# Mask rows for each bit of a hash, made by GpSimd; scores capped in place with their minimum

## What is computed

```python
q_bits = (np.einsum('bhsd,dk->bhsk', q, proj) > 0)      # 6 bits per row
k_bits = (np.einsum('bhsd,dk->bhsk', k, proj) > 0)
mask = q_bucket[:, :, :, None] == k_bucket[:, :, None, :]
scores = np.where(mask, scale * np.matmul(q, k.transpose(0, 1, 3, 2)), -1000000000.0)
attn = np.exp(scores - np.max(scores, axis=-1, keepdims=True))
attn = attn / (np.sum(attn, axis=-1, keepdims=True) + 1e-09)
out = np.matmul(attn, v)
```

## Time and profile before

| what | value |
|---|---|
| median of the runs | 616.49 us (616.34 to 616.92) |
| profiled execution | 616.41 us |
| its span in the trace | 614.7 us |
| TensorE busy | 605.4 us, 98% of the span |
| VectorE busy | 431.1 us, 70% |
| ScalarE busy | 347.6 us, 57% |
| GpSimd busy | 349.3 us, 57% |

### The profile page before, as it was taken

How to read it: one execution, slowest core, us unless ns; L and a number is a source line. 1 busy time by engine, 2 the same in 40 slices (tenths; PEclk the granted TensorE clock), 3 DMA queues, 4 the chain that set the end, 5 groups by cost and what they waited for, 6 DMA issues and landing times.

```text
span 614.7 us, 10917 instructions
## 1 busy us (share of the span) xinstructions
PE 605.4 (98%) x3676; PEld 503.5 (82%) x3676; DVE 431.1 (70%) x689; ACT 347.6 (57%) x700; POOL 349.3 (57%) x337
## 2 busy tenths in 40 slices
PE   7899999999999999999999999999999999999998
PEld 3667777776776776999888999999999999988887
DVE  3988888888888885788676666545677666579920
ACT  3877777777777785354444444335444444264232
POOL 4533434333337756146458988873999999234140
PEclk9999999999999999999999999999999999999999
DMA  6842323233232210001212122113222221100202
GB/s 137 244 118 64 91 66 91 64 90 90 64 90 79 62 46 3 1 2 53 69 51 69 56 64 61 60 57 99 69 85 85 86 86 51 35 1 0 86 19 102
DMA packets 27650, 42.20 MB, mean 69 GB/s; under 512 B 3425, under 2 KB 15713, under 8 KB 27617
## 3 DMA queue, kind: packets, MB, share of 16 engines
q1 hardware_dynamic: 25648, 37.38, 20.9%
q0 software_dynamic: 1728, 4.02, 2.6%
q10 hardware_dynamic: 240, 0.39, 0.3%
HBM read 38.63 MB, written 3.15 MB: 68 GB/s over the span
## 4 chain that ended last, share of the span: by engine, by line
PE 95%; DVE 2%; DMA 1%; ACT 1%; POOL 1%; issue 0%; ACTq 0%; POOLq 0%
PE banks L1882 22%; PE banks L1914 16%; PE banks L1667 12%; PE banks L1684 11%; PE banks L1734 10%; PE banks L1996 5%; PE banks L2012 5%; PE banks L1873 4%; PE banks L1707 2%; PE banks L1818 2%; PE banks L1620 2%; DMA k_raw<-in_k 1%; PE banks L1742 1%; PE banks L1858 1%; PE banks L1626 1%; PE banks L1792 1%
## 5 line engine op out<-in xcount | busy, mean ns | idle before, releaser
L1246 DVE TENSOR_REDUCE row_min<-banks 128x1 f32<-128x768 f32 x96 | 91.8, 956 | 31.8 <-PE banks L1667 31.1
L873 ACT ACTIVATE prob<-banks,row_min 128x768 f32<-128x768 f32 x96 | 87.1, 907 | 29.0 <-DVE row_min L1246 28.9
L1506 DVE TENSOR_TENSOR partial_sums<-banks,partial_sums 128x384 f32<-128x384 f32 x78 | 43.4, 557 | 54.9 <-PE banks L1914 54.7
L1734 PE MATMUL banks<-ident,prob 128*128 128x128 f32 x576 | 79.2, 273 | 1.4 <-ACT probT L374 1.4
L1734 PEld LDWEIGHTS banks<-ident,prob 128*128 128x128 f32 x576 | 68.1, 140 | 6.7 <-issue 1.9
L606 POOL TENSOR_TENSOR k_b<-k_raw,k_a 64x768 fp32r<-64x768 f32 x16 | 29.3, 1829 | 70.7 <-ACT k_a L856 70.7
L1684 PE MATMUL banks<-probT,v_in 128*64 128x384 f32 x384 | 69.0, 494 | 0.0
L1882 PE MATMUL banks<-h_hi,w_hi 128*128 128x512 f32 (+1 forms) x256 | 66.1, 339 | 0.0
L1882 PE MATMUL banks<-h_hi,w_lo 128*128 128x512 f32 (+1 forms) x256 | 65.6, 337 | 0.0
L1882 PE MATMUL banks<-h_lo,w_hi 128*128 128x512 f32 (+1 forms) x256 | 65.3, 336 | 0.0
L374 ACT COPY probT<-banks 128x384 f32<-128x384 f32 x104 | 49.1, 480 | 22.4 <-PE banks L1734 22.1
(11 more groups left out here) (216 smaller groups left out, 1515.0 us busy)
## 6 DMA issues: line engine op xcount, KB each, us to landing
w_stage<-in_moe_w_ch SPq DMA_DIRECT2D x38, 256.0 KB, 2.6
q_raw<-in_q SPq DMA_DIRECT2D x32, 192.0 KB, 3.3
k_raw<-in_k SPq DMA_DIRECT2D x30, 192.0 KB, 3.6
w_pair<-in_moe_w_ch SPq DMA_DIRECT2D x7, 512.0 KB, 3.7
v_in<-in_v SPq DMA_DIRECT2D x16, 192.0 KB, 2.8
w_stage<-in_moe_w_ch SPq DMA_DIRECT2D x6, 512.0 KB, 3.8
out<-y_out SPq DMA_DIRECT2D x11, 256.0 KB, 2.0
seq_tables_sb<-in_dft POOLq DMA_DIRECT2D x6, 386.0 KB, 3.7
```

The source lines that it names most:

```text
L873: act.activation(prob[s % 2][:, :, :], s_tile(s), ACT.Exp, bias=row_min[:, s:s + 1], scale=-1.0, accum_out=row_sum[:, s:s + 1]).then_inc(e ...
L1246: dve.tensor_reduce(row_min[:, s:s + 1], s_tile(s), AX.XY, ALU.min).then_inc(min_ready, 1)
L1506: dve.tensor_tensor(out, product_bank[PRODUCT_BANK[o]], other, ALU.add).then_inc(done, 1)
L1734: op = pe.transpose(bank[:, j * P:(j + 1) * P], prob[tile % 2][:, c, j * P:(j + 1) * P], ident[:, :])
```

## The change

There are no buckets any more. For each of six bits the product of a query row and a key row is 2^44 where the query has the bit and the key has not, and six more rows stand for the other case. So 12 rows in a group of 32 rows replace the 64, and a score gets 2^44 for each bit that differs. C0 and C1 are gone from TensorE and VectorE. VectorE's B now writes bits times 1 (q) or 2^44 (k), and GpSimd makes the mask rows of a head with four subtractions of 32 x 384 (`make_mask`); for the very first head VectorE makes them. The second pair of score matmuls reads 96 rows in place of 128. The minimum becomes an operation that also writes the scores back, capped at 2^44, into their own banks. ScalarE adds the 1e-9 of the denominators, which VectorE did before. VectorE copies P1 out in slot 9 too. In pair 7 ScalarE rounds two parts of the Fourier input in slots 8 and 9 in place of 6 and 7, and GpSimd's folding for it is split around the masks. The last P1 of a pair is put in the second bank.

```diff
-        PREPARE = {0: ["B"], 2: ["C0"], 4: ["C1"], 6: ["B"], 8: ["C0"], 10: ["C1"]}
-        C1_SLOTS = [s for s in sorted(PREPARE) if "C1" in PREPARE[s]]
+        PREPARE = {0: ["B"], 6: ["B"]}
...
-        P1_BY_ACT = (9,)
+        P1_BY_ACT = ()
...
         banks = [n % 3 for n in range(len(uses))]
+        if banks[-1] == banks[0]:
+            banks[-1] = banks[1]
...
-        prologue = ["B", "C0", "C1"]
+        prologue = ["B"]
...
+        def make_mask(eng, h, chunk):
+
+            cols = slice(chunk * HALF, chunk * HALF + HALF)
+            q_rows = slice(chunk * GROUP, (chunk + 1) * GROUP)
+            k_rows = slice(D + chunk * GROUP, D + (chunk + 1) * GROUP)
+            eng.tensor_tensor(q_b[h][MASK_ROWS, cols], bits_sb[q_rows, :],
+                              bit_offset[q_rows, :].broadcast_to([GROUP, HALF]), ALU.subtract).then_inc(mask_ready, 1)
+            eng.tensor_tensor(k_b[h][MASK_ROWS, cols], bit_offset[k_rows, :].broadcast_to([GROUP, HALF]),
+                              bits_sb[k_rows, :], ALU.subtract).then_inc(mask_ready, 1)
...
+            def masks(i, use):
+
+                h, nxt = head_of_task(i, use)
+                wait_drained(pool, i, use)
+                for chunk in range(2):
+                    make_mask(pool, h, chunk)
+                pool.wait_ge(mask_ready, 4 * (operands(i + nxt, h) + 1))
...
             split_qk(0, 0)
+            pool.wait_ge(offset_loaded, 16)
+            masks(0, (0, "B"))
             split_qk(0, 1)
...
             def prepare_pair(i):
 
+                masks(i - 1, (6, "B"))
                 split_qk(i, 0)
                 scale_q(i, 1)
                 at = bass.ds(2 * (i - 1), 2) if not isinstance(i, int) else slice(2 * (i - 1), 2 * i)
                 pool.dma_start(seq_tab[:, at, :], seq_tables[:, at, :]).then_inc(tables_loaded, 16)
+                masks(i, (0, "B"))
                 split_qk(i, 1)
                 scale_q(i + 1, 0)
 
-            with pool.Fori(1, NP - 2) as i:
+            pool.wait_ge(fold_edge, 3)
+            prepare_pair(1)
+            with pool.Fori(2, NP - 2) as i:
                 prepare_pair(i)
             prepare_pair(NP - 2)
 
             wait_drained(pool, PPB, (9, "O"))
...
-            fold_rows(0, slice(0, DM))
+            fold_rows(0, slice(0, DM), (0,))
+            pool.wait_ge(rows_added, HT)
+            masks(NP - 2, (6, "B"))
             split_qk(NP - 1, 0)
             scale_q(NP - 1, 1)
-            pool.wait_ge(fold_edge, 3)
+            fold_rows(0, slice(0, DM), (1,))
+            pool.wait_ge(rows_subtracted, HT)
+            masks(NP - 1, (0, "B"))
+            split_qk(NP - 1, 1)
+            pool.wait_ge(lo_done, 4 * NP)
             fold_first()
             fold_edges(0)
-            split_qk(NP - 1, 1)
...
+            def add_tiny(i, h):
+
+                need(act, exp_done, i * SLOTS + T * (h + 1))
+                need(act, inv_ready, i * 2 + (h - 1))
+                act.activation(row_den[:, h, :], row_sum[:, T * h:T * (h + 1)], ACT.Identity,
+                               bias=tiny[:, 0:1]).then_inc(den_ready, 1)
...
                         softmax_exp(i, s)
+                    if s == 7 and last < 2:
+                        add_tiny(i, 0)
+                    if s == 1 and not (isinstance(i, int) and i == 0):
+                        add_tiny(i - 1, 1)
...
-                    if last == 1 and s in (6, 7):
-                        round_parts(0, s - 6)
+                    if last == 1 and s in (8, 9):
+                        round_parts(0, s - 8)
...
+            dve.wait_ge(consts_ready, 5)
+            twice = proj_sb[:, :].unsqueeze(1).broadcast_to([D, 2, BITS])
+            both = [w[top, 0:2 * BITS].rearrange("p (n c) -> p n c", n=2) for w in (w_q, w_k)]
+            dve.tensor_scalar(both[0], twice, -1.0, None, ALU.mult).then_inc(w_ready, 1)
+            dve.tensor_copy(both[1], twice).then_inc(w_ready, 1)
...
-                op.then_inc(scratch_free[bank_of(i, use)], 1)
+                if not (isinstance(i, int) and i < 0):
+                    dve.wait_ge(mask_ready, 4 * operands(i + nxt, h))
+                dve.tensor_scalar(bits_sb[:, :], scratch(i, use), 0.0, bit_size[:, :], ALU.is_gt, ALU.mult)\
+                   .then_inc(scratch_free[bank_of(i, use)], 1)
 
             def row_minimum(i, s):
 
                 need(dve, scores_done, i * SLOTS + (s + 1))
-                dve.tensor_reduce(row_min[:, s:s + 1], s_tile(s), AX.XY, ALU.min).then_inc(min_ready, 1)
+                dve.tensor_scalar(s_tile(s), s_tile(s), BIG, None, ALU.min, ALU.min,
+                                  accum_out=row_min[:, s:s + 1]).then_inc(min_ready, 1)
 
             def invert_sums(i, h):
 
-                need(dve, exp_done, i * SLOTS + T * (h + 1))
-                sums = row_sum[:, T * h:T * (h + 1)]
-                dve.tensor_scalar(row_den[:, h, :], sums, 1e-9, None, ALU.add).then_inc(inv_step, 1)
-                need(dve, inv_step, i * 4 + (2 * h + 1))
-                dve.reciprocal(row_inv[:, h, :], row_den[:, h, :]).then_inc(inv_step, 1)
+                need(dve, den_ready, i * 2 + (h + 1))
+                dve.reciprocal(row_inv[:, h, :], row_den[:, h, :]).then_inc(inv_ready, 1)
...
-            for task in prologue:
-                prepare(-1, (0, task))
+            prepare(-1, (0, "B"))
+            dve.wait_ge(offset_loaded, 16)
+            wait_drained(dve, -1, (0, "B"))
+            for chunk in range(2):
+                make_mask(dve, 0, chunk)
...
+                    need(pe, mask_ready, 4 * (operands(i, h) + 1))
...
-                for lhs, rhs, start in ((q_a[h], k_a[h], True), (q_b[h], k_b[h], False)):
+                upper = slice(0, D + GROUP)
+                for lhs, rhs, start in ((q_a[h], k_a[h], True), (q_b[h][upper], k_b[h][upper], False)):
...
             prepare(-1, (0, "B"))
-            keep_busy(2)
-            pe.wait_ge(codes_loaded, 16)
-            prepare(-1, (0, "C0"))
-            prepare(-1, (0, "C1"))
-            for blocks in (3, 3):
+            for blocks in (3, 3, 3, 3):
                 keep_busy(blocks)
...
-    number = np.arange(P - dim)
-    has = (number[None, :] >> np.arange(bits)[:, None]) & 1
-    codes = np.zeros((P, 2, P), np.float32)
-    for chunk in range(2):
-        codes[32 * chunk:32 * chunk + bits, chunk, :dim] = 2 * has - 1
-        codes[64 + 32 * chunk:64 + 32 * chunk + bits, chunk, dim:] = 2 * has - 1
-    ones = np.zeros((P, 1), np.float32)
-    ones[:dim, 0] = ones[dim:, 0] = has.sum(axis=0)
-    return codes, ones
+    size, offset = np.ones((P, 1), np.float32), np.zeros((P, 1), np.float32)
+    size[dim:] = 2.0 ** 44
+    for group in range(0, P, P // 4):
+        if group < dim:
+            offset[group + bits:group + 2 * bits] = 1.0
+        else:
+            offset[group:group + bits] = 2.0 ** 44
+    return size, offset
```

83 lines of the change are left out of this document (24 added, 59 removed).

## The result

The changed kernel takes **615.11 us** (median of 20 runs, 613.28 to 616.20) against 616.52 us for the kernel before (20 runs); the ratio is 0.9971 with a 95% interval of 0.9962 to 0.998. That is 1.4 us less, inside the forecast range and 0.7 us above the number. The profiled execution took 615.87 us, with a span of 614.2 us. So the total came out, but it is made of other terms than the forecast's: each later pair gains nearly twice what was predicted, and the start gives most of that back (in the profiled execution 3.0 of 3.5 us).

A forecast was written before the change was run, and what follows sets the result against it. The prediction took TensorE, nearly free of waits between slots, to bound the kernel. Gains of 1.4 us over pairs 1 to 6, 0.5 in the first and 0.1 in pair 7 gave 2.0 off 616.41: 614.4, range 610.5 to 616.6.

The forecast's parts named there:

- The product's 0.17: TensorE, slots 2, 4, 8, 10: each removed C0 or C1 product saves 0.17 us of start-to-start distance, 0.68 a pair.
- The stall of 0.08 in slot 5: TensorE's transposes in slot 5 wait 0.08 us for VectorE's copy of slot 4's P1; this wait goes.
- 0.28 + 3d = 0.52 a pair: New TensorE waits per pair: 0.04 + d each in slots 5 and 11, 0.20 + d for P1 of slot 11.
- d: Extra time of the capped minimum over the plain one, for its accumulator read: 0.08 us, bounds 0 and 0.96.
- 0.20 + d for the copy of slot 9: With this copy on VectorE, P1 of slot 11 waits 0.20 + d for the bank it shares with slot 10.
- for the one who waits and for VectorE alike: The cap delays both the waiting engine and VectorE's own next work by d = 0.08 us.
- The 0.76 taken off: TensorE saves 0.76 us a pair: 0.68 from the removed products and 0.08 from slot 5's stall.
- The first pair, "0.5 won": Start: first scores 0.5 us later, then 0.35 + 0.35 won there and 0.35 in the rest; 0.5 won.
- What was hidden: GpSimd's masks (0.85 us each), splits and scaling end before they are wanted; batch 1 folding slips about 3 us, 1.5 spare.
- VectorE's waits do not bite: Rival, chance 0.21: cap no longer than the minimum, bank free sooner, most of 0.52 a pair stays; 610.4 us.
- The cap at half speed: Rival, chance 0.07: VectorE's cap reads and writes one bank in turn, each minimum 1.77 us; 640 us.
- The masks come late: Rival, chance 0.04: GpSimd's masks, from 2.3 us each, set the head's length; at 2.5 us each, 627 us.

The follow-up runs named there:

- run 11: The changed kernel unchanged, run once more for another trace: 615.82 us.
- run 12: The changed kernel with nine keep-busy TensorE products at the start in place of four, run once more for another trace: 613.94 us.
- run 10: The changed kernel with one bucket-shaped product more ahead of the scores in slots 2, 4, 8 and 10, without drains: 618.53 us.
- run 9: The changed kernel with slot 9's copy of the second halves back on ScalarE, as before the change: 613.62 us.
- run 2: The changed kernel with the first head's masks reading one tensor and a per-partition pointer scalar in place of two tensors: 613.49 us.
- run 3: The changed kernel with the first head's two splits on VectorE behind its masks, so GpSimd is idle there: 613.88 us.
- run 1: The changed kernel with nine keep-busy TensorE products of three blocks at the start in place of four: 615.25 us.
- run 4: The changed kernel with pointer scalars in the first head's masks and seven keep-busy products in place of four: 613.38 us.
- run 5: The changed kernel with pointer scalars in the first head's masks and that head's splits on VectorE: 613.09 us.
- run 8: The changed kernel with the minimum as a plain reduction again, without the cap: 613.74 us.
- run 7: The changed kernel with the masks of every head on VectorE and none on GpSimd: 651.21 us.

## Why the prediction was right, and where its steps were not

The time and its sign came out as forecast, but by luck in part: two errors of opposite sign cancel in good part. By the two traces, from mark to mark (slot 1 of pair 1 at 40.97 and 43.51, slot 1 of pair 7 at 213.99 and 213.89, the Fourier part at 241.61 and 241.12), in us won:

| stretch | forecast | measured |
|---|---|---|
| first pair | 0.5 | -2.5 (-3.0 up to slot 7, 0.45 behind it) |
| pairs 1 to 6 | 1.4 | 2.6 |
| pair 7 | 0.1 | 0.4 |
| sum | 2.0 | 0.5 |

The medians are 1.4 apart; it fits that the changed kernel loses less at the start in part of its executions (runs 11 and 12).

**What bounds the kernel** held: the gain came through TensorE's distances and its few waits, and VectorE's 4.6 us less in 27 gave nothing by themselves: with the products alone put back (run 10) a pair is as long as before.

**The product's 0.17** held where nothing waits: slots 2 and 8 are shorter by 0.18 and 0.17 and run 10 gives the same. In slots 4 and 10 the changed kernel gained 0.05 each from transposes to transposes (1.55 to 1.50, 1.54 to 1.49): the product's 0.17 less the new wait that the forecast had put at 0.12. Run 10 gives 0.06 and 0.07 for the product there. The 0.19 and 0.14 of the table are those 0.05 and the shift of the first row. Nothing is left that VectorE's lost drains would have to explain. The stall of 0.08 in slot 5 went as forecast: transposes to the product with V are 0.75 there now.

**The waits, 0.28 + 3d = 0.52 a pair**, were mis-sized. In slots 5 and 11 the wait for the exponential is 0.10 each, against 0.04 + d = 0.12. The third term, 0.20 + d for the copy of slot 9, came out at 0.04 in the timeline and 0.09 in run 9. The step that failed is "for the one who waits and for VectorE alike": the read of the accumulator lies beside VectorE's next instruction (both at 107.18), so the "d twice" of slot 10 is d not at all. The base of 0.20 was too long as well: slot 10's minimum starts 122.31 - 120.49 = 1.82 behind slot 9's, where the forecast took 1.94 from slots 3 and 4, since the output is divided 0.46 behind the copy instead of 0.58 (in slot 3 of the changed kernel it is 0.58 still; why is open). So of the 0.52 some 0.25 was there, and nearly all that was missing is this one term. The 0.76 taken off, less 0.25, would be 0.51; the pair gained 0.43, since other distances grew by 0.01 to 0.02 each.

"VectorE: DVE Perf Modes", section "Two Vector instructions with no wait between them", of the Trainium skill, says that such an operation is two instructions. The trace agrees (the row of 0.14); that it costs the engine nothing here is the measurement's.

**Net per pair**: 0.43 for the predicted 0.24; over pairs 1 to 6 2.6 us for 1.4. Pair 7 got its 0.23 (229.58 to 230.33 is 0.75, before 0.98), 0.4 in all.

**The first pair, "0.5 won"**, is the step that failed outright: 3.0 us lost in the profiled execution. The forecast had TensorE's keep-busy products as the last to end, at 13.65, and did not price VectorE's four masks at all. At 0.55 each they would have ended at 11.7. Beside GpSimd's splits they ended at 14.67, and the idle TensorE then ran at half speed. Runs 2 and 3 show the first part, runs 1, 4 and 5 the second. In numbers, the first scores started 1.58 later (14.73 for 13.15), half speed cost 1.78 up to slot 7 (14.63 for 12.85), and what the change won there, once the clock held, was 0.37 (12.85 for 13.22) where the forecast counted 0.70. On the first, "Advanced Engine Details and Errata", section "GPSIMD Details", of the Trainium skill has the rule that the forecast missed: GpSimd shares a read and a write interface with VectorE, and conflicts with VectorE instructions that have two SBUF inputs or run in a two-port mode. "VectorE: DVE Perf Modes", section "Mode 2×_2P — use both read ports for one tensor", of the Trainium skill adds that an operation on one SBUF tensor may take both ports to go faster. Run 2 agrees with both: the form with a pointer scalar is shorter (0.41 against 0.55) and is held all the same. The masks of run 3, with nothing beside them, are never held. That it is a port, and not something else the two engines share, no run here shows. The keep-busy products were also costed at one speed only (4.84 us from the earlier trace rows); they took 2.85 to 5.00.

**What was hidden** was: masks of 0.82 on GpSimd, splits and scaling in time, no wait for `mask_ready` behind the first pair. The score matmuls on 96 rows take 0.51 to 0.52 a pair of products, as on 128 rows, so nothing was the right price for them. The fold for batch 1 slipped as counted (238.07, 5.91 long) with 1.5 us left before VectorE's read at 245.50.

**The rivals.** "VectorE's waits do not bite" was half right: its mechanism, a cap no longer for VectorE and a bank free sooner, is what runs 8 and 9 show, and with an unharmed start the kernel goes to 613.1 to 613.4; its 610.4 is not reached, since the waits of 0.10 for the exponentials stay. In slot 11 it was nearly right: the forecast wanted the transposes drawn out by 0.3 to 0.4 there and named "slot 11 shows no wait" as a sign against itself, and the wait was 0.04. The cap at half speed is excluded by 0.964. "The masks come late" happened, though on VectorE in the first head, not on GpSimd, whose 0.82 is far from 2.3.

## What to carry to other kernels

Price the prologue like the loop: an operation that moves there meets other neighbours, and a wait there may cost the clock as well as its own length. Where VectorE has an operation like these masks, from SBUF to SBUF with two tensors or with a tensor and a pointer scalar, beside a GpSimd instruction on two tensors, take the end of that instruction as its earliest end. A product taken from TensorE is worth its distance to the next one where TensorE never waits, and about a third of it in a slot that ends in a wait; put one back to find out which. Before you split a gain between neighbouring slots, check that the rows you count from start alike in both kernels.

## What the runs showed that was not expected

- VectorE on 32 x 384 in SBUF: 0.55 us with GpSimd idle, 1.39 to 2.08 beside a GpSimd operation on two tensors, by how much of it was left (1.98 and 2.05 in the changed kernel); with a pointer scalar 0.41, and 1.33 and 1.93 beside it. VectorE's drains from PSUM in the kernel before, from 10.41 to 12.94 beside the same splits, took 0.61 to 0.62, unharmed.
- `DVE_READ_ACCUMULATOR`: 0.14 us, starts with the following instruction, delays a waiting ScalarE by 0.07 and VectorE by nothing that can be read (0.01).
- The same eight products on TensorE took 2.85 us in some executions and 4.68 to 5.00 in others, while the granted clock of the stretch read 1.00 in both. In these traces idle times of 0.47, 0.64, 0.73 and 1.35 us ahead of the first scores left the clock at 1.00; behind 1.70, 2.03, 2.33 and 3.71 us it fell, to 0.50 to 0.67 in the windows behind them.
- In run 7 single waits of about 2.0 us in the pairs cost the clock in some places and not in others: the product behind took 3.53 to 3.80 us behind 1.99 to 2.08 us of idle time, and 2.16 behind 1.98 to 2.04.
